# Attention scores as three 64-row products, two heads in the two row halves, with whole-tile splits

## The reference, cut

```python
# attention: q, k, v of (2, 8, 768, 64), n_global = 8, n_local = 96
scores = scale * q @ k.T                       # per batch and head
is_global = pos[None, :] < n_global
is_local = (rel >= 0) & (rel < n_local)        # rel = query - key
bias = -slopes[h] * dist                       # dist = n_local on global keys, else |rel|
scores = where(is_global | is_local, scores + bias, -1e9)
a = exp(scores - max) / (sum + 1e-9)
x = a @ v                                      # (2, 768, 512) after joining the heads
# then a token mixer and channel mixer with ReLU (w_tok1, w_tok2, w_ch1, w_ch2),
# then theta = x @ w_theta, x*cos, x*sin mixed over tokens by two 768x768 matrices,
# and a last channel mixer with w_ch
```

## Time and profile before

| | |
|---|---|
| median of 3 runs | 559.53 us (559.32 to 559.75) |
| span of the profiled execution, first to last instruction | 558.8 us (the page gives no other time of it; the median is 0.7 above) |
| busy: PE, PEld, DVE, ACT, POOL | 520.8, 480.2, 296.1, 184.5, 149.8 us |
| attention, by the timeline | to about 116 us |
| mean granted clock of TensorE | 0.979 of full |
| q and k loads | 11 of 1056 KB, 4.9 us to landing |

### The profile page before, as it was taken

One profiled execution on the slowest core, in us unless ns is written; L12 is line 12 of the kernel. 1 busy time (PEld: TensorE's weight loads), 2 busy tenths in 40 slices (PEclk: granted clock), 3 DMA queues, 4 the chain that ended last, 5 costly groups with the idle time before them and its releaser, 6 DMA issues.

```text
span 558.8 us, 8294 instructions
## 1 busy us (share of the span) xinstructions
PE 520.8 (93%) x3060; PEld 480.2 (86%) x3060; DVE 296.1 (53%) x709; ACT 184.5 (33%) x474; POOL 149.8 (27%) x143
## 2 busy tenths in 40 slices
PE   2979978976999999999999999999879999999997
PEld 2869868954899999997999999998768899888887
DVE  5999999866511132116511133418874483756442
ACT  3879888931211112112211113332142231233120
POOL 6656665569600000000400002242800040000040
PEclk9999998986999999999999999999979999999999
DMA  6636564413400000000200001123100002000002
GB/s 249 251 106 247 193 208 140 149 60 114 132 1 1 0 1 1 0 1 0 75 40 0 1 0 57 23 91 96 38 1 0 1 18 82 15 1 1 2 16 97
DMA packets 9262, 35.08 MB, mean 63 GB/s; under 512 B 1152, under 2 KB 3200, under 8 KB 7808
## 3 DMA queue, kind: packets, MB, share of 16 engines
q1 hardware_dynamic: 9216, 34.48, 18.3%
HBM read 31.33 MB, written 3.15 MB: 62 GB/s over the span
## 4 chain that ended last, share of the span: by engine, by line
PE 78%; DVE 14%; issue 5%; ACT 2%; POOL 1%; DMA 1%; DVEq 0%; ACTq 0%
PE bank L261 67%; PE bank L1112 4%; PE bank L1077 2%; DVE wsplit L777 2%; DVE tile L891 2%; DVE scores L850 2%; PE bank L1093 1%; DVE third L891 1%; PE bank L1185 1%; PE bank L1212 1%; DVE gprobs L795 1%; PE bank L1140 1%; DVE wsplit L788 1%; ACT wsplit L668 1%; DVE zb L928 1%
## 5 line engine op out<-in xcount | busy, mean ns | idle before, releaser
L261 PE MATMUL bank<-split,wsplit 128*128 128x384 f32 x768 | 144.0, 339 | 0.8 <-DVE act_raw L1026 0.8
L261 PEld LDWEIGHTS bank<-split,wsplit 128*128 128x128 f32 x768 | 135.2, 188 | 1.0 <-DVE act_raw L1026 1.0
L261 PE MATMUL bank<-hid,wsplit 128*128 128x384 f32 (+1 forms) x648 | 128.3, 346 | 0.0
L261 PEld LDWEIGHTS bank<-hid,wsplit 128*128 128x128 f32 x648 | 115.3, 189 | 3.7 <-DVE hid L959 0.6
L261 PE MATMUL bank<-wsplit,zs 128*128 128x512 f32 (+1 forms) x576 | 105.3, 343 | 0.2 <-DVE zs L941 0.2
L986 DVE SCALAR_TENSOR_TENSOR hid<-bank,hid 128x384 fp32r<-128x384 f32 x48 | 26.8, 557 | 142.9 <-ACT hid L707 142.9
L261 PEld LDWEIGHTS bank<-wsplit,zs 128*128 128x128 f32 x576 | 90.5, 191 | 13.7 <-issue 0.4
L560 POOL TENSOR_TENSOR wsplit<-wraw,wsplit 128x1536 fp32r<-128x1536 f32 (+1 forms) x16 | 52.5, 3279 | 99.5 <-ACT wsplit L668 98.7
L707 ACT ACTIVATE hid<-bank 128x384 fp32r<-128x384 f32 x48 | 23.6, 491 | 151.8 <-PE bank L261 151.8
L629 ACT ACTIVATE probs<-scores,nmax 128x232 f32<-128x232 f32 (+1 forms) x96 | 44.8, 467 | 17.9 <-DVE nmax L850 17.0
L1112 PEld LDWEIGHTS bank<-vt,probsT 128*128 128x128 f32 (+1 forms) x352 | 41.7, 187 | 9.2 <-ACT probsT L582 7.8
(11 more groups left out here) (101 smaller groups left out, 538.5 us busy)
## 6 DMA issues: line engine op xcount, KB each, us to landing
wraw<-weights SPq DMA_DIRECT2D x16, 768.0 KB, 4.2
qk_raw<-qk SPq DMA_DIRECT2D x11, 1056.0 KB, 4.9
vt<-v SPq DMA_DIRECT2D x12, 256.0 KB, 2.6
out<-act_raw SPq DMA_DIRECT2D x16, 192.0 KB, 1.9
wraw<-weights SPq DMA_DIRECT2D x4, 512.0 KB, 3.5
qk_raw<-qk SPq DMA_DIRECT2D x1, 792.0 KB, 5.3
vg<-v_first SPq DMA_DIRECT2D x2, 256.0 KB, 5.3
qk_raw<-qk SPq DMA_DIRECT2D x1, 264.0 KB, 3.4
```

Source lines behind the costliest of these rows:

```text
L261: mm = pe.matmul(dst, lhs(a), rhs(c), start=first and i == 0, stop=last and i == 2, skip_group_check=True)
```

## The change

The operands of the scores are stacked by pairs of heads: head 2p in the upper 64 partitions, head 2p + 1 in the lower. hi and lo are separate tiles. A step's scores are three products of 64 rows for each head, in the order hi*hi (both heads), hi*lo (both), lo*hi (both), each head in its own row half and its own PSUM bank. The bytes of q and k halve. The ring of key places is gone (six tiles are kept). The splits are done for a whole tile of all heads, at p = 1 of the unit before: ACT rounds queries and keys, DVE subtracts both; POOL has no part in it. POOL splits the four weight chunks beside the attention in whole pieces of 1536 columns, as they arrive. q and k have three buffers and a DMA each, two tiles ahead.

```diff
-RING = 4
-PLACES = [0, 1, 2, 3, 1, 2]
+QBUFS = 3
...
-BESIDE = [0, 1, 4, 7]
-SLICES = 3
+BESIDE = 4
...
-        qk_raw = sb("qk_raw", [P, 2, H, P + KW], F32, attn_mem)
+        q_in = sb("q_in", [P, QBUFS, PAIRS, P], F32, attn_mem)
+        k_in = sb("k_in", [P, QBUFS, PAIRS, KW], F32, attn_mem)
...
+                if n >= QBUFS:
+                    sp.wait_ge(q_lo, n - QBUFS + 1)
+                    sp.wait_ge(k_lo, n - QBUFS + 1)
+                sp.dma_start(q_in[:, n % QBUFS], qk[b, t, :, :, 0:P]).then_inc(q_landed[n % QBUFS], 16)
+                sp.dma_start(k_in[:, n % QBUFS], qk[b, t, :, :, P:]).then_inc(k_landed[n % QBUFS], 16)
...
+                if n + QBUFS - 1 < UNITS:
+                    load_queries_keys(n + QBUFS - 1)
+                if n % 2 == 0 and n // 2 < BESIDE:
+                    load_weight(n // 2)
...
+            def split_weight(i):
+                slot, width = ORDER[i] % SLOTS, WIDTHS[ORDER[i]]
+                raw = wraw[:, i % 2, 0:width]
+                pool.wait_ge(w_in[i % 2], 16 * (i // 2 + 1))
+                link(pool.tensor_copy(w_at(slot, 0, 0, width), raw))
+                pool.tensor_tensor(w_at(slot, 1, 0, width), raw, w_at(slot, 0, 0, width).bitcast(F32),
+                                   ALU.subtract).then_inc(w_ready, 1)
+
+            for i in range(BESIDE):
+                split_weight(i)
...
+            def queries_keys_hi(n):
+                b, t = divmod(n, T)
+                act.wait_ge(q_landed[n % QBUFS], 16 * (n // QBUFS + 1))
                 if n >= 2:
                     act.wait_ge(s_ready, 2 * PAIRS * (n - 1))
+                act.activation(q_split[:, n % 2, 0], q_in[:, n % QBUFS], ACT.Copy).then_inc(q_hi, 1)
+                act.wait_ge(k_landed[n % QBUFS], 16 * (n // QBUFS + 1))
+                act.activation(k_split[:, 0, :, t * KW:(t + 1) * KW], k_in[:, n % QBUFS],
+                               ACT.Copy).then_inc(k_hi, 1)
...
                 if 2 <= m < STEPS + 2:
                     take_pT(m - 2)
-                if n + 1 < UNITS:
-                    keys_hi(n + 1, p)
+                if p == 1 and n + 1 < UNITS:
+                    queries_keys_hi(n + 1)
...
+            def queries_keys_lo(n):
+                cols = slice(n % T * KW, (n % T + 1) * KW)
+                dve.wait_ge(q_hi, n + 1)
+                dve.tensor_tensor(q_split[:, n % 2, 1], q_in[:, n % QBUFS], q_split[:, n % 2, 0].bitcast(F32),
+                                  ALU.subtract).then_inc(q_lo, 1)
+                dve.wait_ge(k_hi, n + 1)
+                dve.tensor_tensor(k_split[:, 1, :, cols], k_in[:, n % QBUFS],
+                                  k_split[:, 0, :, cols].bitcast(F32), ALU.subtract).then_inc(k_lo, 1)
...
-            split_first(0)
             for h in range(H // 2):
                 dve.tensor_scalar(bias[:, h, :], c_base, SLOPES[h], None, ALU.mult).then_inc(bias_ready, 1)
-            split_first(1)
+            queries_keys_lo(0)
...
                 if m >= 2:
                     gather(m - 2)
-                if m == 0:
-                    for later in range(2, PAIRS):
-                        split_first(later)
-                if n + 1 < UNITS:
-                    queries_hi(n + 1, p)
-                if 1 <= m <= STEPS - PAIRS:
-                    keys_lo((m - 1) // PAIRS + 1, (m - 1) % PAIRS)
+                if p == 1 and n + 1 < UNITS:
+                    queries_keys_lo(n + 1)
...
-                for e in range(2):
-                    h = 2 * p + e
-                    for i in range(2):
-                        mm = pe.matmul(S_BANK[m % 2][e][:, first:WIN], q_split[:, n % 2, h, :],
-                                       k_split[:, i, h, keys], start=i == 0, stop=i == 1)
-                    mm.then_inc(s_ready, 1)
+                for i, (x, y) in enumerate(((0, 0), (0, 1), (1, 0))):
+                    for e in range(2):
+                        rows = slice(e * D, (e + 1) * D)
+                        mm = pe.matmul(S_BANK[m % 2][e][:, first:WIN], q_split[rows, n % 2, x, p, :],
+                                       k_split[rows, y, p, keys], start=i == 0, stop=i == 2)
+                        if i == 2:
+                            mm.then_inc(s_ready, 1)
```

More of the change, by code:

```diff
@@ L173, in build @@
         bias_ready = sem("bias_ready")
-        pair_in = sem("pair_in")
-        qk_in = [sem(f"qk_in{i}") for i in range(2)]
+        q_landed = [sem(f"q_landed{i}") for i in range(QBUFS)]
+        k_landed = [sem(f"k_landed{i}") for i in range(QBUFS)]
         v_in = [sem(f"v_in{i}") for i in range(3)]
+        gathered = sem("gathered")
+        q_hi = sem("q_hi")
         k_hi = sem("k_hi")
-        q_hi = sem("q_hi")
+        q_lo = sem("q_lo")
         k_lo = sem("k_lo")
-        q_lo = sem("q_lo")
-        gathered = sem("gathered")
         vg_in = sem("vg_in")
@@ L263, in three @@
             return mm
-        def places(t):
-            return [PLACES[t]] if t != RING - 1 else [RING - 1, 0]
-        def splits(n, p=PAIRS - 1):
-            return PAIRS * sum(len(places(i % T)) for i in range(n)) + (p + 1) * len(places(n % T))
         UNITS = B * T
@@ L582, in take_pT @@
                 act.activation(dst, src, ACT.Copy).then_inc(pT_taken, 1)
-            def keys_hi(n, p):
-                heads = slice(2 * p, 2 * p + 2)
-                if n == 0 and p == 0:
-                    act.wait_ge(pair_in, 16)
-                else:
-                    act.wait_ge(qk_in[n % 2], 16 * (n // 2 + 1))
+            def queries_keys_hi(n):
+                b, t = divmod(n, T)
+                act.wait_ge(q_landed[n % QBUFS], 16 * (n // QBUFS + 1))
                 if n >= 2:
                     act.wait_ge(s_ready, 2 * PAIRS * (n - 1))
-                for place in places(n % T):
-                    act.activation(k_split[:, 0, heads, place * KW:(place + 1) * KW],
-                                   k_in[:, n % 2, heads], ACT.Copy).then_inc(k_hi, 1)
+                act.activation(q_split[:, n % 2, 0], q_in[:, n % QBUFS], ACT.Copy).then_inc(q_hi, 1)
+                act.wait_ge(k_landed[n % QBUFS], 16 * (n // QBUFS + 1))
+                act.activation(k_split[:, 0, :, t * KW:(t + 1) * KW], k_in[:, n % QBUFS],
+                               ACT.Copy).then_inc(k_hi, 1)
             def global_probsT(n):
@@ L607, in global_values_hi @@
                 act.activation(vg_split[:, 0], vg[:, :], ACT.Copy).then_inc(vg_hi, 1)
-            keys_hi(0, 0)
+            queries_keys_hi(0)
             act.wait_ge(base_ready, 1)
@@ L612, in _ @@
                 act.activation(bias[:, h, :], c_base, ACT.Copy, scale=SLOPES[h]).then_inc(bias_ready, 1)
-            for p in range(1, PAIRS):
-                keys_hi(0, p)
             for m in range(STEPS + 3):
@@ L771, in _ @@
             dve.wait_ge(base_ready, 1)
-            def keys_lo(n, p):
-                heads = slice(2 * p, 2 * p + 2)
-                for i, place in enumerate(places(n % T)):
-                    dve.wait_ge(k_hi, splits(n, p) - len(places(n % T)) + i + 1)
-                    cols = slice(place * KW, (place + 1) * KW)
-                    dve.tensor_tensor(k_split[:, 1, heads, cols], k_in[:, n % 2, heads],
-                                      k_split[:, 0, heads, cols].bitcast(F32), ALU.subtract).then_inc(k_lo, 1)
-            def queries_hi(n, p):
-                heads = slice(2 * p, 2 * p + 2)
-                if n == 0 and p == 0:
-                    dve.wait_ge(pair_in, 16)
-                else:
-                    dve.wait_ge(qk_in[n % 2], 16 * (n // 2 + 1))
-                if n >= 2:
-                    dve.wait_ge(s_ready, 2 * PAIRS * (n - 1))
-                dve.tensor_copy(q_split[:, n % 2, heads], q_in[:, n % 2, heads]).then_inc(q_hi, 1)
+            def queries_keys_lo(n):
[6 more added lines that the diff above has]
+                                  k_split[:, 0, :, cols].bitcast(F32), ALU.subtract).then_inc(k_lo, 1)
             def gather(m):
```

97 lines of the change are left out of this document (27 added, 70 removed).

## The result

The kernel after takes 595.36 us, median of 4 (591.19, 593.10, 597.62, 621.25); the kernel before took 559.64 beside it (559.32 to 561.32). The ratio is 1.060 (95% interval 1.055 to 1.066): slower by 6%, where 567.0 in a range of 553 to 580 was forecast. The direction was right, the size was not. The profiled execution is the one of 591.19 us; its span is 589.4.

The account below looks back on a forecast made before the run. DVE first, with TensorE and ACT close, was taken to bound the attention. Units 1 to 11 at 90.2, POOL 7.5, clock 1 gave 98.7 against 94.1 (+4.6); unit 0 +3: +7.6, forecast 567.0 us, range 553 to 580.

Parts of the forecast that it names:

- 1 for the clock: Attention, units 1 to 11: long gaps lower TensorE's clock, costing 1 us; mean clock was 0.98 before.
- 8.2 a unit: Attention: TensorE's sum for a clean unit of 128 queries, four steps, taken as the pace: 8.2 us.
- TensorE's step: Attention, two heads: scores 0.60 and two passages of 0.09 bring the step from 1.66 to 1.91 us.
- the forecast's lower bound of three pitches (0.40): Scores of a step: six 64-row products fully side by side take 0.40 us, a gain of 0.13.
- the passages: TensorE's two changes per step between 128-row and 64-row work: 0.09 us each, bounds nothing and 0.27.
- DVE's wait for ACT: At p = 1 of each unit, DVE's subtractions wait for ACT's rounding: 1.75 us of 3.05 a unit.
- DVE's 7.45: Attention: DVE's sum for a unit, its wait for ACT included, 7.45 us; 8.15 with a bias copy.
- Unit 0, +3: First attention unit: POOL's first weight delays DVE's splits, so unit 1's first scores come 3 us later, about 20.4.
- POOL, 2.5 exposed a weight: Attention: POOL's whole-tile weight splits hold DVE 3.4 us a weight, 2.5 exposed; three weights behind unit 0 cost 7.5.
- The fast one (553.5): Rival: row halves side by side, cheap passages, no DVE wait, ACT bounds units at 6.95 us; 553.5 us, chance 0.19.
- The slow one (584): Rival: each passage costs a whole matmul, 0.27 us, step 2.47, unit 10.5; +24, 584 us, chance 0.12.
- The second (563): Rival: DVE's wait is the bound alone, TensorE below 7.4 a unit; +4 over units 1 to 11, 563 us, chance 0.21.

Follow-up runs that it names:

- experiment 1: Kernel after with its six score matmuls a step on 128 rows instead of 64, both heads' scores summed: 582.38 us, ratio 1.037.
- experiment 2: Kernel before with its four 128-row score matmuls a step made six 64-row ones, nothing else: 590.76 us, median of four.
- 14: Kernel after with splits by pairs of heads, POOL's weight pieces in thirds, and six 128-row score matmuls, both heads summed: 555.63 us, ratio 0.992.
- 11: Kernel after with splits by pairs of heads, and three score products of one head, then three of the other: one execution, 585.96 us.
- Experiment 6: Kernel after, complete, with splits by pairs: ACT rounds one pair of heads each step, DVE subtracts it one step later: 592.27 us.
- Experiment 3: Kernel after, complete, with DVE's whole-tile subtractions moved one step later, behind the global rest and the inverse sums: 596.18 us.
- 9: Kernel after with splits by pairs and four 128-row score matmuls a step, third product left out, heads summed: 564.34 us, ratio 1.007.
- 10: Kernel after with splits by pairs, four 128-row score matmuls (third product out, heads summed) and POOL's weight pieces in thirds: 552.01 us, ratio 0.985.
- 13: Kernel after, complete, with splits by pairs and POOL's weight pieces in thirds, six 64-row score products kept: 568.81 us, ratio 1.006.
- 5: Kernel after with four 128-row score matmuls a step, third product left out and both heads summed: 580.00 us, ratio 1.035.
- 12: Kernel after with splits by pairs and two extra 128-row matmuls per step whose results nobody reads: 583.98 us, ratio 1.041.

## Why the prediction was wrong

Two terms of the sum failed, and one of them alone would have taken the time out of the range.

**"1 for the clock" failed.** It measured about 18 more than before, by the split above. The mean of 0.98 over the stage was carried over to a TensorE list that no row of before has. Experiments 1, 2 and 14 change the rows of the score products and show it, at the medians: +30 where 64-row products are put alone into the kernel before, -13 where they are taken out, once with the stalls there and once with the splits repaired. The falls come behind stalls: in the kernel after the clock falls behind POOL's third and fourth weight, when DVE stood 3.16 us beside POOL's subtraction (first two rows below) and TensorE waited 2.86 us in the end. Its timeline:

```profile
66.77 3.44 POOL L507 TENSOR_TENSOR wsplit<-wraw,wsplit 128x1536 fp32r<-128x1536 f32 x1
67.08 3.16 DVE L760 TENSOR_SCALAR rinv<-psum 128x8 f32<-128x8 f32 x1
```

```profile
72.48 1.00 PE L1059 MATMUL bank<-vt,probsT 128*128 128x64 f32 x8 [2.86 <-ACT probsT L555]
...
97.22 0.33 PE L1077 MATMUL bank<-ident,gprobs 128*128 128x128 f32 x1 [1.56 <-DVE gprobs L755]
```

Then a list with 64-row products stayed low for 10 to 58 us (but 6.8 in 11), busy 93 to 100% of it, where the kernel before and experiment 1 came back in 3.4 to 6.8. What could have been read: the kernel before lost 3.4 us at the low clock behind one stall, and there were to be four long ones. That warned of more than 1, though not of 18. No rival had the clock in it.

**"8.2 a unit" failed: 9.05.** Its two halves went apart. TensorE's step was forecast at 1.91 and is 1.80, in part by luck: the scores, taken at 0.60 because the loads were thought to overlap in part only, run fully side by side, at the forecast's lower bound of three pitches (0.40), and the passages cost some 0.13 each and not 0.09. The two misses partly cancel. DVE's wait for ACT was forecast at 1.75 and is 1.65. Both sums came near; the way in which they were put together was wrong. I took the larger of two engine sums, TensorE's 8.2 and DVE's 7.45, as the unit. But the three engines hang in one loop of waits: DVE stands until ACT has rounded, TensorE's global product stands behind DVE's L773, which lies behind that lump, and the values behind ACT's copy. So 1.2 us of the lump come on top of 7.8. Experiment 6 shows it: with the splits by pairs the unit is 7.78, the TensorE sum 4 x 1.80 + 0.57 = 7.77. Experiment 3 shows that the place of the lump matters little.

**Unit 0, +3: right in mechanism and nearly in size.** The third step's reduction was forecast at 19.4 and came at 18.59, unit 1's scores at 20.4 and came at 21.18, which is +3.8. The timeline of the kernel after, answering to the earlier trace rows:

```profile
14.35 3.74 POOL L507 TENSOR_TENSOR wsplit<-wraw,wsplit 128x1536 fp32r<-128x1536 f32 x1
14.73 3.93 DVE L747 TENSOR_TENSOR wsplit<-k_in,wsplit 128x544 fp32r<-128x544 f32 x1
18.59 0.28 DVE L801 CUSTOM_DVE_ANT_0 scores<-bank,bias 128x136 f32<-128x136 f32 x1
```

The subtraction of 0.72 took 3.93 and ended 0.57 behind POOL's, as the earlier trace rows had it. The rest of the delay is in TensorE's list: unit 1's scores stand behind the values of an earlier step, which waited for ACT's copy until 20.13 and took 1.05 at the low clock.

**POOL, 2.5 exposed a weight.** Where TensorE is not slow itself (9 against 10), whole pieces cost 12 us for four weights, 3 each, falls of the clock included. In the kernel after, TensorE's waits beside the second, third and fourth weight are 3.10, 2.86 and 1.56 us, together the 7.5 of the forecast; what was missing is the low clock behind them.

**The rivals.** The fast one (553.5) asked for a unit below 7.7 with ACT as the bound. Its premise on the row halves came true: the pairs start 3 ns apart. The Trainium skill (TensorE: Matmul & The Clock Gate, Part 3) says that matmuls in distinct row groups run at once, and the trace agrees. But with the passages TensorE alone stands at 7.8, DVE did wait for ACT, and the clock fell. The slow one (584) wanted 0.27 for each passage; it is some 0.13. The Trainium skill (TensorEngine Tiling, Key Properties) has each change of the tiling mode drain TensorE; the trace agrees in so far as time is lost at the two changes, 0.25 us a step. 584 would have been nearer in time, for a wrong reason. The second (563) took DVE's wait as the bound alone; the wait came as forecast, but on top of TensorE's sum.

Put together with the measured terms: 11 x 9.05 = 99.6, the clock 21, the remainder 2, so 122.6 against the forecast's 98.7; with unit 0 3.8 and -1.6 behind the attention the span is 589.4 (the remainder was set so). The median lies another 4 us higher, as the executions' clock differs. One reading of the prediction is off without effect: DVE stands at 8 or 9 in seven of the first eight slices, not six.

**What stays open.** What decides when the clock falls and rises. The rows of the products matter (13 and 14), and falls come behind stalls. But the edit from 64 to 128 rows also ends the running side by side and the passages, and no experiment parts these three. And 5 was low twice for 17 us with 128-row products, and 12 was low for 55 us with extra ones. Why the same kernel goes from 573 to 612 us (experiment 6) is not explained either; the profile shows only how long the low stretch was.

## What to carry to other kernels

Before operands are packed so that a matmul uses fewer rows, price TensorE's clock, not only the matmuls: here the packed products cost 6 us at full clock and, at the median of four runs, 24 more through the low clock (experiment 2). Judge such a version by several runs: these four lay between 573 and 609 us. Whether small products run side by side is read from their single starts and not from the time of the whole group: here they did, and the passages ate the gain. A wait on one engine is added to the bound of another, and not hidden beside it, when the engines wait for one another within two steps; spread a whole-tile lump over the steps. And a long elementwise instruction on POOL is charged to DVE in whole: cut it where DVE has work beside it.

## What the runs showed of the hardware

- Two 64-row products of fp32r in different row halves start 3 ns apart; a pair of 232 columns follows the other at 0.11 us, the distance of two single 128-row products. This holds also where the list has three of one half and then three of the other (10 ns apart, experiment 11).
- Going from 128-row to 64-row work and back cost about 0.25 us a step together, an estimate from steps of 1.80 and 1.66. So six 64-row products take 0.53 us to the next transpose, as four of 128 rows do; six of 128 rows take 0.75.
- With 64-row products in the list, TensorE stayed at 1.2 GHz for 58 us at 99% busy (experiment 2).
- The granted clock of a window ahead of the first recorded change reads 1.00 although the matmuls' lengths show the low clock, here for 49 us. The mean clock of such an execution looks better than it was: the one of experiment 11 has a mean of 0.977, though its matmuls are at the low length to 86 us (it took 585.96 us).
- A DVE instruction on 8 columns (L760, 0.17 alone) took 3.16 beside POOL's subtraction of 1536 columns. The Trainium skill (SBUF — State Buffer, Who interferes with whom) has the two engines share a port pair that one of them holds for its whole instruction; the trace agrees, with 3.16 to 3.93 us.
